# Last down blocks of the first layer among the second layer's steps, and waits by bank

## The reference

```python
# linear attention: B, H, S, D = 4, 8, 768, 48
for t in range(S):
    cur = einsum('bhd,bhe->bhde', u * k_t, v_t)
    y[:, :, t] = einsum('bhd,bhde->bhe', r_t, state + cur)
    state = w * state + einsum('bhd,bhe->bhde', k_t, v_t)
x = y.transpose(0, 2, 1, 3).reshape(3072, 384)
x = (silu(x @ w_gate) * (x @ w_val)) @ w_out            # layer 1, 384 -> 1536 -> 384
xn = x / sqrt(mean(x * x) + 1e-6) * rms_g
return (silu(xn @ w_gate2) * (xn @ w_val2)) @ w_out2    # layer 2, own weights
```

## Time and profile before

| | us |
|---|---|
| median of 3 runs | 995.81 (994.24 to 995.89) |
| the profiled execution | 995.4, span 993.5 |
| TensorE matmuls, busy | 964.3 (97%), 9426 of them |
| TensorE weight loads, busy | 797.2 (80%) |
| VectorE, GpSimd, ScalarE, busy | 679.7, 549.4, 404.3 |
| mean granted TensorE clock | 0.986 |

### The profile page before, as it was taken

The page is one execution under the profiler, slowest core; times in us unless marked ns, Lnnn a source line. Parts: engine busy times, 40 slices in busy tenths (PEclk is TensorE's granted clock), DMA queues, the critical chain, the costliest instruction groups (busy, mean ns, idle before and its releaser), DMA issues.

```text
span 993.5 us, 23903 instructions
## 1 busy us (share of the span) xinstructions
PE 964.3 (97%) x9426; PEld 797.2 (80%) x9426; DVE 679.7 (68%) x1074; ACT 404.3 (41%) x851; POOL 549.4 (55%) x441
## 2 busy tenths in 40 slices
PE   7989999999999999999999999999999999999998
PEld 5989988888888888888877777787888777878876
DVE  4786756576857756674419967788677799567760
ACT  4544343334333433433432454434633446344423
POOL 7598876566666565565233315678526787211134
PEclk7899999999999999999999999999999999999999
DMA  7554443535434343533142155443064441344201
GB/s 296 163 172 127 147 135 116 180 105 182 174 125 149 131 149 112 175 144 124 56 154 85 43 187 216 159 154 111 33 223 157 140 160 53 105 171 159 80 1 64
DMA packets 50495, 134.58 MB, mean 135 GB/s; under 512 B 6800, under 2 KB 10320, under 8 KB 50384
## 3 DMA queue, kind: packets, MB, share of 16 engines
q1 hardware_dynamic: 50384, 133.05, 38.7%
HBM read 106.78 MB, written 25.17 MB: 133 GB/s over the span
## 4 chain that ended last, share of the span: by engine, by line
PE 75%; POOL 7%; DVE 7%; issue 7%; DMA 1%; ACT 1%; POOLq 0%; SPq 0%; DVEq 0%; ACTq 0%
PE ps_down L883 7%; PE ps_down L885 6%; PE ps_down L884 6%; PE ps_val L883 6%; PE ps_val L885 6%; PE ps_val L884 6%; PE ps_gate L883 5%; PE ps_gate L885 5%; PE ps_gate L884 5%; PE ps_level L979 4%; PE ps_level L1184 2%; PE ps_level L1186 2%; PE ps_level L1185 2%; PE ps_val L1184 1%; PE ps_val L1044 1%
## 5 line engine op out<-in xcount | busy, mean ns | idle before, releaser
L1964 POOL TENSOR_TENSOR h_lo<-h_raw,h_hi 128x512 fp32r<-128x512 f32 (+1 forms) x84 | 113.2, 1348 | 220.4 <-ACT h_hi L1291 211.6
L883 PE MATMUL ps_down<-h_hi,down_hi 128*128 128x512 f32 (+1 forms) x360 | 134.9, 375 | 1.7 <-DVE room_c L1818 0.9
L885 PE MATMUL ps_down<-h_lo,down_hi 128*128 128x512 f32 (+1 forms) x360 | 132.6, 368 | 0.0
L884 PE MATMUL ps_down<-h_hi,down_lo 128*128 128x512 f32 (+1 forms) x360 | 132.6, 368 | 0.0
L1567 DVE TENSOR_TENSOR h_raw<-h_raw,ps_val 128x512 f32<-128x512 f32 (+1 forms) x84 | 51.0, 608 | 88.0 <-PE ps_val L885 79.9
L1291 ACT ACTIVATE h_hi<-h_raw 128x512 fp32r<-128x512 f32 (+1 forms) x84 | 47.9, 571 | 150.1 <-DVE h_raw L1567 150.0
L883 PE MATMUL ps_gate<-x_hi,up_weights 128*128 128x512 f32 (+1 forms) x252 | 94.7, 376 | 1.6 <-ACT h_raw L1285 1.6
L883 PE MATMUL ps_val<-x_hi,up_weights 128*128 128x512 f32 (+1 forms) x249 | 91.1, 366 | 4.2 <-DVE h_raw L1567 2.5
L885 PE MATMUL ps_gate<-x_lo,up_weights 128*128 128x512 f32 (+1 forms) x252 | 91.7, 364 | 0.0
L884 PE MATMUL ps_gate<-x_hi,up_weights 128*128 128x512 f32 (+1 forms) x252 | 91.5, 363 | 0.0
L885 PE MATMUL ps_val<-x_lo,up_weights 128*128 128x512 f32 (+1 forms) x249 | 90.0, 362 | 0.0
(11 more groups left out here) (293 smaller groups left out, 2402.7 us busy)
## 6 DMA issues: line engine op xcount, KB each, us to landing
ring<-sums_dram SPq DMA_DIRECT2D x72, 640.0 KB, 4.8
r_block<-in_r_blk_dram SPq DMA_DIRECT2D x22, 768.0 KB, 5.1
chunk_in<-in_a_t_dram SPq DMA_DIRECT2D x24, 512.0 KB, 3.7
chunk_in<-in_a_n_dram SPq DMA_DIRECT2D x22, 384.0 KB, 4.3
sums_dram<-sum_lo SPq DMA_DIRECT2D x24, 320.0 KB, 3.1
staging<-in_weights_dram SPq DMA_DIRECT2D x18, 384.0 KB, 3.9
raw<-in_blocks_dram SPq DMA_DIRECT2D x8, 576.0 KB, 5.5
sums_dram<-sum_hi SPq DMA_DIRECT2D x12, 320.0 KB, 2.6
```

The source lines that it names most:

```text
L883: nc.tensor.matmul(dst, w_hi, x_h, start=first, stop=False)
L884: nc.tensor.matmul(dst, w_lo, x_h, start=False, stop=False)
L885: return nc.tensor.matmul(dst, w_hi, x_l, start=False, stop=last)
L1964: nc.gpsimd.tensor_tensor(h_lo[:, f % 3, 0:WIDTH[t]], h_raw[:, f % 2, 0:WIDTH[t]], h_hi[:, f % 3, 0:WIDTH[t]].bitcast(F32), ALU.subtract). ...
```

## The change

- The last two down blocks of the last tile (f = 10, 11; `LATE` = 2) leave the end of layer 1. Their six parts stand among the steps of triple 0 of round 0, behind steps 11, 15, 15, 25, 25, 27.
- Their result is copied out, bank by bank, behind `copy_part` at steps 8, 9, 10 of triple 1 of round 0, and the `copy_out2(r, 1)` of the other rounds goes from step 3 to the same steps. SyncE stores the last tile in the middle of triple 1, and the next x load waits for one store less.
- A down part of the first block waits for its own bank alone, the copy of it (n = 0) or the last add from it (n = 1), and not for all three. The parts of (1, 0, 0) go in the order in which their banks come free.
- The last nine parts go block by block for the first two banks, then the third bank.
- The last piece of the second layer's down weights gets its own place, over weights that the last up product has used, and is loaded behind the ring loads. ScalarE splits it at step 14 of triple 1, GpSimd behind its third `split_h2` there.

```diff
+LATE = 2
+LATE_AT = (11, 15, 15, 25, 25, 27)
+COPY_OUT_AT = (8, 9, 10)
+LAST_DOWN2_AT = 14
...
+def bank_left(r, part):
+    b = down_banks(r, 1)[part]
+    chains = BANKS[r][TRIPLES - 1]
+    if b == chains[4]:
+        return adds(r, TRIPLES - 2, STEPS - 1)
+    return adds(r, TRIPLES - 1, 2 * PRODUCT.index(CHAINS[chains.index(b) // 2][-1]) + chains.index(b) % 2)
+
+def parts(r, n, q, m):
+    return sorted(range(KT), key=lambda part: bank_left(r, part)) if (n, q, m) == (1, 0, 0) else list(range(KT))
...
+        down2_last = over("down2_last", [P, PIECE], F32, "up_weights", 4 * 4 * PIECE + (FT - 2) * TOK)
...
             def load_down2(p):
...
+                if p == PAIRS - 1:
+                    sp.wait_ge(up_done, TILES1 * 2 * FT)
+                sp.dma_start(down2_from(p), down2[p]).then_inc(down2_loaded[p % 2], 16)
...
             def load_x2(k):
...
-                    if r == 1 and n == 0:
-                        sp.wait_ge(out_stored, 16 * stores(TILES1))
+                    if n == 0:
+                        sp.wait_ge(out_stored, 16 * stores(TILES1 - 1 if r == 1 else TILES1))
...
-                if g < PAIRS - 2:
+                if g < PAIRS - 3:
                     load_down2(g + 2)
-            store(TILES1 - 1)
+            load_down2(PAIRS - 1)
...
                     if r and g % GROUPS == 8:
                         store2(r - 1, 1)
+                    elif g == 8:
+                        store(LAST)
...
             def down2_part(r, n, q, m, part):
-                if part == 0:
+                if part == parts(r, n, q, m)[0]:
                     pe.wait_ge(h_hi_done, u + 1)
                     pe.wait_ge(h_lo_done, u + 1)
...
-                    if f == 0 and n == 0:
-                        pe.wait_ge(out_copied, (TILES1 + 2 * r) * KT)
-                    elif f == 0:
-                        pe.wait_ge(part_added, adds(r, TRIPLES - 1, STEPS - 1))
+                if f == 0 and n == 0:
+                    pe.wait_ge(out_copied, (TILES1 + 2 * r - 1) * KT + part + 1)
+                elif f == 0:
+                    pe.wait_ge(part_added, bank_left(r, part))
...
-                    if not 0 < t <= AHEAD or s > 0:
+                    if (not 0 < t <= AHEAD or s > 0) and not (t == LAST and s >= SLOTS - LATE):
                         group(t, kind, f)
...
+                        for i, at in enumerate(LATE_AT):
+                            if (r, q, s) == (0, 0, at):
+                                down_part(LAST, FT - LATE + i // KT, i % KT)
...
                 for n, q, m in BETWEEN:
-                    for part in range(KT):
+                    for part in parts(r, n, q, m):
                         down2_part(r, n, q, m, part)
-            for part in range(KT):
+            for several in (range(KT - 1), [KT - 1]):
                 for n, q, m in BEHIND:
-                    down2_part(ROUNDS - 1, n, q, m, part)
+                    for part in several:
+                        down2_part(ROUNDS - 1, n, q, m, part)
...
-                copy_out(t)
+                if t < LAST:
+                    copy_out(t)
...
-                        if r and q == 1 and s == 3:
-                            copy_out2(r - 1, 1)
+                        for m in range(KT):
+                            if q == 1 and s == COPY_OUT_AT[m] and r:
+                                copy_out2(r - 1, 1, [m])
+                            elif q == 1 and s == COPY_OUT_AT[m]:
+                                copy_out(LAST, [m])
+                        if r == 0 and q == 1 and s == LAST_DOWN2_AT:
+                            split_down2(PAIRS - 1)
...
+                        if r == 0 and q == 1 and i == 2:
+                            split_down2(PAIRS - 1)
```

More of the change, by code:

```diff
@@ L522, in build, with down2_from @@
                      over("room_d", [P, TOK], F32, "chunk_in", (2 * FREED + 2) * TOK)[:, :])
+        down2_last = over("down2_last", [P, PIECE], F32, "up_weights", 4 * 4 * PIECE + (FT - 2) * TOK)
+        def down2_from(p):
+            return down2_last[:, :] if p == PAIRS - 1 else staging[:, p % 2, :]
         def val_room(r, q, out):
@@ L751, in load_down2 @@
                 if p >= 2:
-                    if p % 2:
+                    if p == PAIRS - 1:
+                        pass
+                    elif p % 2:
                         sp.wait_ge(down2_lo_pool, p // 2)
@@ L759, in load_down2 @@
                     sp.wait_ge(sums_stored[1], 16 * GROUPS)
-                sp.dma_start(staging[:, p % 2, :], down2[p]).then_inc(down2_loaded[p % 2], 16)
+                if p == PAIRS - 1:
+                    sp.wait_ge(up_done, TILES1 * 2 * FT)
+                sp.dma_start(down2_from(p), down2[p]).then_inc(down2_loaded[p % 2], 16)
             def load_ring(g):
@@ L906, in end_val, with down_part @@
                 last.then_inc(up_done, 1)
+            def down_part(t, f, m):
+                n, W = t * FT + f, WIDTH[t]
+                if m == 0:
+                    pe.wait_ge(h_hi_done, n + 1)
+                    pe.wait_ge(h_lo_done, n + 1)
+                c = (f % 2) * DM + m * P
+                last = three_terms(ps_down[:, m, 0:W], down_hi[:, f // 2, c:c + P], down_lo[:, f // 2, c:c + P],
+                                   h_hi[:, f % 3, 0:W], h_lo[:, f % 3, 0:W], f == 0, f == FT - 1)
+                if m == KT - 1:
+                    last.then_inc(down_done, 1)
             def group(t, kind, f):
@@ L917, in group @@
                 if kind == "down":
-                    pe.wait_ge(h_hi_done, n + 1)
-                    pe.wait_ge(h_lo_done, n + 1)
                     if f == 0 and t == 0:
@@ L925, in group @@
                     for m in range(KT):
-                        c = (f % 2) * DM + m * P
-                        last = three_terms(ps_down[:, m, 0:W], hi[:, f // 2, c:c + P], lo[:, f // 2, c:c + P],
-                                           h_hi[:, f % 3, 0:W], h_lo[:, f % 3, 0:W], f == 0, f == FT - 1)
-                    last.then_inc(down_done, 1)
+                        down_part(t, f, m)
                     return
@@ L1206, in down2_part @@
                     last.then_inc(part_summed, 1)
-                elif part == KT - 1:
+                elif part == parts(r, n, q, m)[-1]:
                     last.then_inc(down_done, 1)
@@ L1300, in split_down2 @@
                 act.wait_ge(down_done, LAST * FT + 2 * p + 2)
-                nc.scalar.activation(down_hi[:, p, :], staging[:, p % 2, :], ACT.Copy).then_inc(down2_hi, 1)
+                nc.scalar.activation(down_hi[:, p, :], down2_from(p), ACT.Copy).then_inc(down2_hi, 1)
             def copy_blocks(u):
@@ L1322, in split_x, with copy_out @@
                 nc.scalar.activation(x_hi[:, kt, 0:WIDTH[t]], x_raw[:, kt, 0:WIDTH[t]], ACT.Copy).then_inc(x_hi_done, 1)
-            def copy_out(t):
+            def copy_out(t, several=range(KT)):
                 reach(act, out_stored, 16 * stores(t))
                 act.wait_ge(down_done, t * FT + FT)
-                for m in range(KT):
+                for m in several:
                     nc.scalar.activation(x_out[:, m, 0:WIDTH[t]], ps_down[:, m, 0:WIDTH[t]], ACT.Copy).then_inc(out_copied, 1)
@@ L1419, in copy_part @@
                         act.wait_ge(down2_lo_dve, PAIRS // 2)
-                        act.wait_ge(down2_lo_pool, PAIRS // 2)
+                        act.wait_ge(down2_lo_pool, PAIRS // 2 - 1)
                     place = val_room(r, q, out)
@@ L1439, in split_h2, with copy_out2 @@
                 nc.scalar.activation(h_hi[:, u % 3, :], h_of(r, q, 2 * m + n), ACT.Copy).then_inc(h_hi_done, 1)
-            def copy_out2(r, n):
+            def copy_out2(r, n, several=range(KT)):
                 act.wait_ge(out_stored, 16 * (stores(TILES1) + 2 * r + n))
                 act.wait_ge(down_done, turn_of(r, n, TRIPLES - 1, 2 if n else 1) + 1)
-                for m in range(KT):
+                for m in several:
                     nc.scalar.activation(x_out[:, m, :], bank[down_banks(r, n)[m]], ACT.Copy).then_inc(out_copied, 1)
@@ L1497, in _ @@
                             split_piece(j)
-                    for p in range(PAIRS):
+                    for p in range(PAIRS - 1):
                         if t == LAST and DOWN2_HIGH[p] == s:
@@ L1577, in split_down2 @@
                 dve.wait_ge(down2_hi, p + 1)
-                nc.vector.tensor_tensor(down_lo[:, p, :], staging[:, p % 2, :], down_hi[:, p, :].bitcast(F32), ALU.subtract)\
+                nc.vector.tensor_tensor(down_lo[:, p, :], down2_from(p), down_hi[:, p, :].bitcast(F32), ALU.subtract)\
                   .then_inc(down2_lo_dve, 1)
@@ L1974, in split_down2 @@
                 pool.wait_ge(down2_hi, p + 1)
-                nc.gpsimd.tensor_tensor(down_lo[:, p, :], staging[:, p % 2, :], down_hi[:, p, :].bitcast(F32), ALU.subtract)\
+                nc.gpsimd.tensor_tensor(down_lo[:, p, :], down2_from(p), down_hi[:, p, :].bitcast(F32), ALU.subtract)\
```

(2 more changed lines are left out.)

## The result

The changed kernel took **984.48 us** (median of 6 runs, 984.24 to 987.29), the kernel before, on the same chip, 995.24 (6 runs, 993.28 to 996.58): ratio 0.990, 95% interval 0.9884 to 0.9915. I had said 987.5 and a range of 985.4 to 990.6: faster, but the median lies 0.9 us under the range.

What follows compares the result with a forecast made beforehand. TensorE was taken to bound the kernel, leaving only idle time between its weight loads to win. Terms 3.1 + 2.9 + 0.85 + 1.1 = 8.0 us took the profiled 995.4 to 987.4, forecast 987.5, range 985.4 to 990.6.

Steps and rivals of the forecast that it cites:

- Late blocks, 3.1: First triple of round 0: six late down parts cover waits for VectorE's adds and ScalarE's copies; gain 3.1 us.
- rival 1: First triple of round 0: VectorE limits it and the six parts add to its waits; 3.1 us less, 990.6; chance 0.06.
- Round ends, 2.9: Behind each round's last step: waiting part by part removes the wait for the last add; gain 0.9 + 0.9 + 1.15.
- what is late next: the third block needs an h_lo: Third block behind the last step: waits for GpSimd's h_lo, so 0.25 us comes back in rounds 0 and 1.
- Rival 2: Round ends: the third block's h_lo keeps TensorE waiting in rounds 0 and 1; 1.8 us less, 989.3; chance 0.07.
- Copies, 0.85: Round 2, triple 1: output copies move from step 3 to steps 8, 9, 10, ending step 8's wait; gain 0.85 us.
- last nine parts, 1.1: End of layer 2: the last block's first part comes fifth, not third, so its h_lo is done; gain 1.1 us.
- rival 3: New place of the copies: one part in each round waits 0.99 us; 3.0 less, 990.5; chance 0.05.
- Newton steps, no cost: Round 0's next norm on GpSimd: Newton steps end between 630.8 and 633.2, up to 0.6 us late, covered; cost nothing.
- the second cover that I named: VectorE after reaching the Newton result: idle for 2.38 us before its next add at 639.47, taken to absorb lateness.
- Rival 4: Late Newton steps on GpSimd hold up VectorE and triple 2's adds; 21.7 us lost, 1009; chance 0.02.
- The sum, 8.0: Whole kernel: gains of 3.1, 2.9, 0.85 and 1.1 us add to 8.0; chance 0.80.

Runs made afterwards that it cites:

- e4_late_only: The kernel before with only the late down blocks, the moved last down piece and the moved copies of layer 1's result: 992.08 us, ratio 0.9973.
- e2_ends: The kernel before with only the round-end part: bank-by-bank waits and the new order of (1, 0, 0)'s parts: 990.61 us, ratio 0.9958.
- e3_all_but_late: The changed kernel without the late down blocks, the last down piece's own place and the late store: 988.1 us, ratio 0.9934.
- e7_newton_later: The changed kernel with GpSimd repeating the split of the last down piece twice ahead of round 0's Newton steps: 993.18 us (one run).
- e8_norm_late: The changed kernel with the norm of each round's second x tile multiplied in at step 11 of triple 3, not step 6: 989.37 us.
- e6_before_raw_early: The kernel before with the first load of raw second-layer weights issued in slot 25, not 33: 996.23 us, ratio 0.9995.

## Why the prediction was right and where it failed

**Late blocks, 3.1: right.** 3.20 in the profile and in the same stretch of `e4_late_only`, 3.34 in the whole layer 2 of the latter, where the copies of the first layer's result are moved too. VectorE kept up (rival 1 is out), and the two gaps left, 0.29 and 0.28, are the ones forecast at 0.2 and 0.15.

**Round ends, 2.9: the mechanism right, the term too small; it measured 3.4** (3.3 in `e2_ends`). The step "what is late next: the third block needs an h_lo" came as forecast, 0.28 us more than a dense distance before the third block in rounds 0 and 1. What I had not counted is that a gap as long goes elsewhere: the kernel before lost 0.25 us before the last of the twelve blocks, at 711.22, and this has gone. Rival 2 is out.

**Copies, 0.85, and last nine parts, 1.1: right**, 0.90 and 1.13. In `e2_ends`, which leaves the copies where they were, the wait is still in triple 1 of round 2 (27.58 us), in `e3_all_but_late` it is gone (26.67). No part waited for a copy at its new place; rival 3 is out.

**Newton steps, no cost: right, by wrong reasons.** I put their end between 630.8 and 633.2 and VectorE's arrival at 632.62. The trace has 629.00 and 629.48. The steps did not begin later by the clock, since the first triple's gain had let GpSimd finish the h_lo ahead of them sooner and the split fell into that time; and VectorE came 3.14 us sooner, as everything on TensorE's path did. Against the triples the steps moved back by 3.2 us (from 613.98 - 603.41 = 10.6 to 614.00 - 600.23 = 13.8 after the start of triple 1). The room between their end and `norm_x` shrank from 3.64 us to 0.48. And the second cover that I named, 2.38 us of idle VectorE, is worth 1.0: `e7_newton_later` shows it. Had the steps come some 1.5 us later (0.48 + 1.0, an estimate from these traces), TensorE would have paid. Rival 4's mechanism is real. It took 3.6 and 2.4 us off its lateness as room; the room was 3.6 and 1.0, of which the change used 3.2. Its price didn't fall due. The sum had no term either for what the clock adds to a wait of TensorE, 1.07 us behind one of 3.76 in `e7_newton_later`. Comparing two absolute times of the kernel before, when the change itself moves one of them, was the mistake. The product of 1.78 us in the earlier trace rows that I put beside Newton steps stands beside an h_lo, as said under `e8_norm_late`; nothing of the sum hangs on it.

**The sum, 8.0: 8.6**, by 0.5 at the round ends and 0.1 at the first triple.

**The range failed at its low end.** The step was "with 1 us for the spread of the runs (994.24 to 995.89) the low end is 985.4". Three runs had shown 1.65 us. The kernel before ran from 992.05 to 999.49 in later measurements, and the changed one from 983.41 to 989.91 in the 17 usable runs of three measurements, with medians of 984.48, 988.58 and 984.83; its lowest run is 8.6 under the lowest of before. Of the 3.0 us between the forecast of 987.5 and the median, 0.6 are the sum; 2.3 are the distance of the median from the profiled execution (986.8), on whose like the forecast was built, and which was the second longest of its six.

In the profiles nearly all of that spread lies in layer 1, which the change hardly touches: 5.1 us in the stretch of 33.9 to 38.9 us, as TensorE pauses there or not and as the clock falls behind the pause or not, and 3.6 us before it. That the two profiles agree at 575.4 was luck. Both have the 1.04 us pause, but so has `e6_before_raw_early`, which begins layer 2 at 574.17.

The runs that left no trace left their granted clock, and it sorts them. Of the 17 of the changed kernel, six had 0.987 or less and took 986.8 to 989.91 (median 988.0); eleven had 0.988 or more and took 983.41 to 986.94 (984.5). Of the 46 of the kernel before that have a clock, 28 and 18 fell into the same two groups, with medians of 996.1 and 994.3. Like with like the change is worth 8.1 and 9.8 us, which brackets the 8.6 of layer 2. Why the first two medians differ by 10.8, some 2 us more, is argued and not shown: four of the changed kernel's six were in the faster group, and the kernel before was there in 18 runs of 46, but of its first six only the profiled one has its clock on record (0.986). A low end of 986.4 less half of a 5 us spread, 984, would have held the median; that spread was measured only later.

**What stays open:** what makes the instruction packet late by up to 2 us in one run and not in another, why the clock's low stretches in the first 75 us differ, why the changed kernel had its lower values more often in two measurements and not in the third, and how the boundaries lie in the program. That TensorE waits for the packet is read from the even distance of 1.2 to 1.45 us between landing and resumption; no view names the wait itself.

## What to carry to other kernels

Measure an edit on the stretch that it touches, from one marked instruction to another: here that repeats to 0.3 us where the time of the whole kernel wanders over 6, and it lets parts of a change be added up.

A wait by part, or filler moved between steps that wait, gives back the gap; ask for each what was next to be late, and for each cover whether the change itself moves one of its two ends. Idle time of an engine is cover only if what ends it does not itself wait for the late work: look for the first reader of the late result on any engine, here ScalarE. And look at the granted clock behind a wait of TensorE before the whole loss is put down to the wait.

The spread of three runs is no bound for the spread of a kernel: look for a stretch whose length differs between profiles of the same program before giving the range its ends, and read the granted clock of every run.

## What the hardware showed that I had not expected

TensorE can stand still inside a run of products that wait for nothing, 0.76 to 2.06 us, at the same instruction in nine of ten profiles; with 24 products added 140 us earlier this pause was gone and another of 1.22 us stood 90 us later. In all eleven cases the loads went on 1.2 to 1.45 us after a 16 KB instruction packet had landed. Where the granted clock fell behind the pause, large loads went at 0.43 us and not at 0.23 for 3.4 us, in `e7_newton_later` for 6.8.
